# Seven block products for eight in the second product of a mixture layer's first stage, with one group of low parts made on GpSimd

## The chip, the core and the metric

The kernel runs on one core of one Trainium2 chip. The metric is the device time of one launch in microseconds, the median over several runs. The engines are TensorE (PE, with its weight loads listed as PEld), VectorE (DVE), ScalarE (ACT) and GpSimd (POOL); SyncE (SP) issues most transfers.

## The reference

Three stages follow each other. A retention layer gives 1536 tokens of 512 features. Layer 1 normalises them and passes them through a gated hidden layer of 1536. Layer 2 adds four experts of hidden size 1024, weighted by normalised probabilities.

```python
x = attn_out.transpose(0, 2, 1, 3).reshape(B * S, H * D)      # 1536 x 512
# layer 1
xn = x / sqrt(mean(x * x) + 1e-6) * rms_g
g, val = xn @ w_gate, xn @ w_val                                # 512 x 1536 each
x = (g * sigmoid(g) * val) @ w_out                              # 1536 x 512
# layer 2
p = domain_probs / (domain_probs.sum(-1, keepdims=True) + 1e-9)
out = sum(p[:, e:e + 1] * (maximum(x @ w1[e], 0) @ w2[e]) for e in range(4))
```

The product that the change touches is the last one of layer 1, hidden values times `w_out`.

## The kernel before

**Precision.** Every operand of a product is split into a high part (rounded to the format fp32r) and a low part (the rest, `raw - high`), and one product of two operands is three matmuls, high x high, low x high and high x low (`three`, L518 to L522).

**Tiling.** The tokens are two sets `j` of 768, each in two halves `a` of 384 (`TB`). A *unit* `q` is one pair of hidden blocks (gate and value, or two hidden blocks of an expert) for one set: a 2x2 block product of `x` (halves of the tokens, halves of the 512 features) with a 2x2 arrangement of weights. It is done with seven block products instead of eight (`PRODUCTS`, in the order M1, M5, M6, M2, M7, M4, M3), each two times three matmuls of 384 columns. Sums of weight blocks (`w_op`) and their parts are made on POOL, sums of token blocks on DVE or POOL. M6, M7 and M4 go on adding in the PSUM bank of M1, so ACT copies the bank after M1, M6 and M7 (`copy_up`), and the next of these products waits for the copy. DVE then forms the four results (`c11`, `c22_sum`, `c12`; the fourth lies in the bank).

**Layer 1** has 24 units (`Q1`), 12 hidden blocks for each of two sets. `silu` (ACT) and `hidden` (DVE, L975) make gate times value for the token half a=1 and then for a=0. In the kernel before, ACT rounds each (`hidden_hi`) into `h1_hi`, DVE subtracts (`hidden_lo`) into `h1_lo`, and four slots of these are held.

**The second product before.** For each pair of hidden blocks and each set (12 *rounds*; round r uses units 2r and 2r+1) there are eight tiles (`tile1`): four blocks of 128 output features times two token halves, each two hidden blocks times three matmuls of 384 columns. They go in turn to PSUM banks 6 and 7, and DVE adds each to `x_all` (`post1`, L1025). Tile n waits until tile n-2 is posted. The tiles are set by hand between the seven products of the two units that follow the round (`FIRST`, `SECOND`: how many at three places of a unit).

**Layer 2** has units of the same kind with `relu_hi`/`relu_lo` and output tiles `tile2`/`post2` of six matmuls of 512 columns. It is not changed but for addresses and for the units that overlap layer 1's last round.

**Queues.** The order of the work on each engine is written out by hand; each engine takes its queue in order, and semaphores with constant counts join them. DVE's order for a unit of layer 1 is posts, `c11`, posts, `c22_sum`, posts, `hidden(q,1)`, `c12`, `hidden(q,0)`, and two `hidden_lo`. POOL's order for one pair of blocks is `split_w(2p)`, `split_w(2p+1)`, `split_wd(p)`: for `w`, four sums of 256 elements a partition, one rounding of 1792 and seven subtractions of 256. `split_w_hi(c)` waits for the last unit that uses block c-2.

Of the kernel before, what the change touches and what calls it, by code (L numbers as in the profile page):

```python
# [32 lines left out]
J = 2  # L33
# [20 lines left out]

F1 = FF1 // P
# [29 lines left out]
def tiles_before(d):  # L85

    if d < F1 // 2:
        return 2 * T1N * (d + 1)
    return T1N * F1 + T2N * (last_unit(F1 + d - F1 // 2) - Q1 + 1)


def h_count(q):

    return 2 * q if q < Q1 else 2 * Q1 + 4 * (q - Q1)


def build(nc, qkv, wu, wd, small, t_y_decay, out):
# [3 lines left out]
    with ExitStack() as ctx:  # L101
        ctx.enter_context(nc.sbuf_tensor("arena", [P, 207 * 256 - 256], F32))

        def sem(name):
            return ctx.enter_context(nc.semaphore(name))

        X_HI, X_LO, ACC, W_RAW, W_HI, W_LO, WD, HH, HL, TMP, OWN = (
            o * KB for o in (17, 38, 101, 125, 133, 147, 161, 177, 189, 201, 219))
# [10 lines left out]
        wd_hi = [at(f"wd_hi{i}", [P, 2, DM], F32R, WD + 8 * KB * i) for i in range(2)]  # L119
        wd_lo = [at(f"wd_lo{i}", [P, 2, DM], F32R, WD + 8 * KB * i + 4 * KB) for i in range(2)]  # L120
        wd_raw = [at(f"wd_raw{i}", [P, 2, DM], F32, WD + 8 * KB * i + 4 * KB) for i in range(2)]
        h1_hi = at("h1_hi", [P, SLOTS1, 2, TB], F32R, HH)
        h1_lo = at("h1_lo", [P, SLOTS1, 2, TB], F32R, HL)
        h2_hi = at("h2_hi", [P, SLOTS2, 2, 2, TB], F32R, HH)
        h2_lo = at("h2_lo", [P, SLOTS2, 2, 2, TB], F32R, HL)
# [9 lines left out]
        y_decay = at("y_decay", [P, 2, DM], F32, HH)  # L135
        y_first = at("y_first", [P, DM], F32, TMP + 12 * KB)
        state = at("state", [P, B, PAIRS * DH], F32, HH + 4 * KB)
        guess = at("guess", [P, 2, TB], F32, HH + 6 * KB)
        guess_sq = at("guess_sq", [P, 2, TB], F32, HH + 9 * KB)
        squares = [at("squares0", [P, SPB, KT, CH], F32, WD + 8 * KB), at("squares1", [P, SPB, KT, CH], F32, HL + 6 * KB)]  # L140
# [51 lines left out]
        w_ready = sem("w_ready")  # L192
        wd_hi_ready = sem("wd_hi_ready")
# [47 lines left out]
        def _(sp):  # L241
# [33 lines left out]
            for p in range(1, F1 // 2):  # L275
# [22 lines left out]
        def _(pool):  # L298
# [88 lines left out]
            for n in range(NSTEP):  # L387
# [884 lines left out]
```

## Time and profile before

| | before |
|---|---|
| median of 3 runs | 844.63 us (844.29 to 844.9) |
| time of the profiled execution | 845.3 us |
| its span | 843.5 us |
| TensorE busy | 832.0 us (99%) |
| VectorE busy | 469.2 us (56%) |
| GpSimd busy | 408.1 us (48%) |
| ScalarE busy | 242.7 us (29%) |
| granted TensorE clock | 1.00 |

A busy share says how much of the span an engine had an instruction at work. TensorE's matmuls overlap, so the mean duration of one (335 ns) is longer than the distance between two; the work is counted by that distance. In the timelines a row is the start, the duration, the engine, the line and the operation, and in brackets the idle time before it and what ended it. A row with x2 or more covers neighbouring instructions together.

### The profile page before, as it was taken

How to read it: one execution, taken by the hardware profiler on the slowest of the kernel's cores; microseconds unless marked ns; L12 is line 12 of the kernel's file. 1: busy time of each engine (PE TensorE's matmuls, PEld its weight loads, DVE VectorE, ACT ScalarE, POOL GpSimd, SP SyncE). 2: the span in 40 equal slices, each digit the busy share in tenths (PEclk: the TensorE clock that was granted, in tenths of full speed). 3: DMA queues.
4: the chain of work that ended last, by engine and by line, in shares of the span. 5: the costliest groups of instructions: out<-in, count | busy, mean ns of one | idle time of the engine just before them, and what ended most of it. 6: DMA issues, size and time to landing. Idle time of an engine off the chain costs nothing.

```text
span 843.5 us, 12814 instructions
## 1 busy us (share of the span) xinstructions
PE 832.0 (99%) x4846; PEld 770.9 (91%) x4846; DVE 469.2 (56%) x776; ACT 242.7 (29%) x483; POOL 408.1 (48%) x460
## 2 busy tenths in 40 slices
PE   8999999999999999999999999999999999999998
PEld 7888999999999998889899989889899898898997
DVE  4698455545555558774554554545545545545545
ACT  2676222222322325422222222222212212222221
POOL 3998835546372739832836336336326325425100
PEclk9999999999999999999999999999999999999999
DMA  9801010100110010101101100110110110110003
GB/s 343 319 33 51 26 51 26 51 26 26 33 44 26 26 51 26 51 1 51 51 8 44 51 13 38 51 31 21 51 40 10 51 51 2 51 51 1 25 14 137
DMA packets 12876, 43.15 MB, mean 51 GB/s; under 512 B 1425, under 2 KB 1809, under 8 KB 12817
## 3 DMA queue, kind: packets, MB, share of 16 engines
q1 hardware_dynamic: 12528, 41.69, 14.0%
q8 instruction: 40, 0.66, 0.3%
q10 hardware_dynamic: 288, 0.65, 0.2%
q14 instruction: 20, 0.16, 0.1%
HBM read 39.19 MB, written 3.15 MB: 50 GB/s over the span
## 4 chain that ended last, share of the span: by engine, by line
PE 93%; POOL 2%; DMA 1%; DVE 1%; ACT 1%; issue 1%; SPq 0%; DVEq 0%
PE bank L520 30%; PE bank L521 30%; PE bank L522 30%; DMA ring<-qkv 1%; PE bank L469 1%; PE bank L462 1%; PE bank L449 1%; PE bank L499 1%; POOL w_lo L342 1%; POOL x_lo L237 0%; ACT x_hi L706 0%; DVE x_sum L233 0%; POOL wd_lo L361 0%; PE bank L482 0%; POOL squares L310 0%
## 5 line engine op out<-in xcount | busy, mean ns | idle before, releaser
L520 PE MATMUL bank<-x_hi,w_hi 128*128 128x384 f32 x784 | 263.9, 337 | 3.1 <-DVE x_lo L237 0.9
L522 PE MATMUL bank<-x_lo,w_hi 128*128 128x384 f32 x784 | 262.8, 335 | 0.0
L521 PE MATMUL bank<-x_hi,w_lo 128*128 128x384 f32 x784 | 262.8, 335 | 0.0
L1041 DVE SCALAR_TENSOR_TENSOR out_acc<-bank,p_norm,out_acc 128x512 f32<-128x512 f32 (+1 forms) x181 | 135.0, 746 | 127.7 <-PE bank L522 127.3
L520 PEld LDWEIGHTS bank<-x_hi,w_hi 128*128 128x128 f32 x784 | 147.2, 188 | 10.9 <-issue 5.5
L521 PEld LDWEIGHTS bank<-x_hi,w_lo 128*128 128x128 f32 x784 | 147.2, 188 | 5.5
L522 PE MATMUL bank<-wd_lo,h_hi 128*128 128x512 f32 (+1 forms) x386 | 152.0, 394 | 0.0
L521 PE MATMUL bank<-wd_hi,h_lo 128*128 128x512 f32 (+1 forms) x386 | 151.6, 393 | 0.0
L520 PE MATMUL bank<-wd_hi,h_hi 128*128 128x512 f32 (+1 forms) x386 | 149.9, 388 | 0.6 <-DVE out_acc L1037 0.3
L522 PEld LDWEIGHTS bank<-x_lo,w_hi 128*128 128x128 f32 x784 | 147.1, 188 | 0.0
L342 POOL TENSOR_TENSOR w_lo<-w_raw,w_hi 128x256 fp32r<-128x256 f32 x196 | 142.8, 762 | 3.0 <-ACT w_hi L678 0.8
L354 POOL TENSOR_SCALAR wd_hi<-wd_raw 128x1024 fp32r<-128x1024 f32 x21 | 22.1, 1053 | 213.5 <-DMA wd_raw<-wd 213.5
L711 ACT ACTIVATE u<-bank 128x384 f32<-128x384 f32 x112 | 55.1, 492 | 200.4 <-PE bank L522 200.3
L335 POOL TENSOR_SCALAR w_hi<-w_raw 128x1792 fp32r<-128x1792 f32 x26 | 44.4, 1707 | 126.4 <-PE bank L522 125.7
L313 POOL TENSOR_TENSOR w_raw<-w_raw 128x256 f32<-128x256 f32 x112 | 83.0, 763 | 19.9 <-DMA w_raw<-wu 17.7
L729 ACT ACTIVATE h_hi<-bank 128x384 fp32r<-128x384 f32 x96 | 47.3, 493 | 138.7 <-PE bank L522 64.8
L522 PEld LDWEIGHTS bank<-wd_lo,h_hi 128*128 128x128 f32 x386 | 72.4, 188 | 15.2
L520 PEld LDWEIGHTS bank<-wd_hi,h_hi 128*128 128x128 f32 x386 | 72.5, 188 | 13.1 <-issue 1.5
L521 PEld LDWEIGHTS bank<-wd_hi,h_lo 128*128 128x128 f32 x386 | 72.4, 188 | 11.9
L999 DVE SCALAR_TENSOR_TENSOR h_lo<-bank,h_hi 128x384 fp32r<-128x384 f32 x96 | 53.2, 554 | 43.6 <-ACT h_hi L729 43.6
L959 DVE TENSOR_TENSOR bank<-bank,m 128x384 f32<-128x384 f32 x56 | 31.6, 565 | 71.2 <-PE bank L522 71.2
L520 PE MATMUL bank<-h_hi,wd_hi 128*128 128x384 f32 x192 | 64.3, 335 | 1.1 <-DVE x_all L1025 1.1
(71 smaller groups left out, 874.5 us busy)
## 6 DMA issues: line engine op xcount, KB each, us to landing
w_raw<-wu SPq DMA_DIRECT2D x28, 512.0 KB, 4.3
ring<-qkv SPq DMA_DIRECT2D x23, 512.0 KB, 9.1
wd_raw<-wd SPq DMA_DIRECT2D x22, 512.0 KB, 3.5
out<-out_acc SPq DMA_DIRECT2D x11, 256.0 KB, 2.0
ring<-qkv ACTq DMA_DIRECT2D x1, 512.0 KB, 7.3
y_first<-t_y_decay SPq DMA_DIRECT2D x1, 256.0 KB, 8.0
out<-out_acc SPq DMA_DIRECT2D x2, 128.0 KB, 1.8
small_sb<-small ACTq DMA_DIRECT2D x1, 126.0 KB, 5.2
```

The source lines that it names most:

```text
L313: return nc.gpsimd.tensor_tensor(w_raw[:, WS[to], :, :], w_raw[:, WS[a], :, :], w_raw[:, WS[b], :, :], ALU.subtract).then_inc(w_sums, 1)
L335: nc.gpsimd.tensor_scalar(w_hi[c % 2][:, :, :, :], w_raw[:, 0:7, :, :], 1.0, 1.0, ALU.mult, ALU.mult).then_inc(w_hi_ready, 1)
L342: nc.gpsimd.tensor_tensor(w_lo[c % 2][:, WS[ws], :, :], w_raw[:, WS[ws], :, :], w_hi[c % 2][:, WS[ws], :, :].bitcast(F32), ALU.subtract).t ...
L354: nc.gpsimd.tensor_scalar(wd_hi[i][:, :, :], wd_raw[i][:, :, :], 1.0, 1.0, ALU.mult, ALU.mult).then_inc(wd_hi_ready, 1)
L520: pe.matmul(dst, s_hi, m_hi, start=first, stop=False, skip_group_check=True)
L521: pe.matmul(dst, s_lo, m_hi, start=False, stop=False, skip_group_check=True)
L522: return pe.matmul(dst, s_hi, m_lo, start=False, stop=last, skip_group_check=True)
L711: nc.scalar.activation(tile[:, s, :], bank[3 * s][:, 0:TB], ACT.Copy).then_inc(u_copied, 1)
L729: nc.scalar.activation(h2_hi[:, q % 2, v, a, :], src, ACT.Relu).then_inc(hi_ready, 1)
L959: nc.vector.tensor_tensor(bank[3 * s + 2][:, 0:TB], bank[3 * s + 2][:, 0:TB], m1[:, s, :], ALU.add).then_inc(c11_ready, 1)
L999: nc.vector.scalar_tensor_tensor(out=h2_lo[:, q % 2, v, a, :], in0=src, scalar=0.0, in1=h2_hi[:, q % 2, v, a, :].bitcast(F32), op0=ALU.max ...
L1041: nc.vector.scalar_tensor_tensor(out=to, in0=new, scalar=p, in1=to, op0=ALU.mult, op1=ALU.add).then_inc(posted, 1)
```

## The change

The hidden values of a round become a 2x2 block operand of their own: token halves a by the two hidden blocks v of units 2r and 2r+1. `w_out`'s two blocks by two halves of 256 features are the other operand. Seven products (`DOWNS`: M2, M1, M6, M7, M4, M5, M3) of two 128-feature tiles each replace the eight tiles: 14 tiles of three matmuls instead of eight of six. M6, M7, M4 add on in the banks of M1, and M3 in those of M5; the banks are posted after every product, so there are 14 posts a round instead of eight, and each tile waits for the post of tile n-2 as before.

`hidden` writes to SBUF (`h1_raw`, `h1_a21`). DVE makes four sums of hidden blocks (`hidden_sum`), ACT rounds them in four groups (one, two, two and two blocks of 384), and DVE subtracts for groups 0, 1 and 2; GpSimd does so for group 3 (S1 and S4) in rounds 0 to 9, and DVE in rounds 10 and 11. GpSimd makes four sums, one rounding of 1792 and seven subtractions of 256 for each `w_out` block pair, where it had one rounding of 1024 and two subtractions of 512. At the start ACT and DVE take these parts of the first block pair. The places of the tiles and the orders of all queues are new. The hidden operands take the place of the four slots in SBUF, and the second hidden buffer of layer 2 lies over them, so its first write waits for layer 1's last tile. `dynamic_dma_scratch_size=2048` is given to the program and the arena grows from 206 KB to 221 KB a partition.

```diff
+DOWNS = (("M2", "A12", "B21", True, ((0, 0),)), ("M1", "A11", "B11", True, ((0, 0),)),
+         ("M6", "S2", "T2", False, ((1, 0),)), ("M7", "S3", "T3", False, ((1, 1),)),
+         ("M4", "A22", "T4", False, ((0, 1),)), ("M5", "S1", "T1", True, ((1, 1),)),
+         ("M3", "S4", "B22", False, ((1, 0),)))
+HS = {"A12": 0, "A11": 1, "S2": 2, "S3": 3, "A22": 4, "S1": 5, "S4": 6}
+GROUPS = (slice(0, 1), slice(1, 3), slice(3, 5), slice(5, 7))
...
-T1N = 2 * KT
+T1N = 2 * NP
...
-FIRST, SECOND = (0, 1, 2), (2, 1, 2)
-EARLY, LATE = (0, 0, 2), (2, 2, 2)
-END0, END1 = (0, 2, 2), (2, 1, 1)
-NEXT0, NEXT1 = (0, 1, 2, 2), (3, 0, 0, 0)
+FIRST, SECOND = (0, 0, 0, 2, 2, 2, 0), (0, 2, 2, 2, 2, 0, 0)
+EARLY, LATE = (0, 0, 0, 0, 2, 2, 2), (0, 2, 2, 2, 2, 0, 0)
+END0, END1 = (0, 0, 0, 2, 2, 2, 2), (2, 2, 0, 0, 2, 0, 0)
+NEXT0, NEXT1 = (0, 0, 0, 0, 2, 2, 2), (2, 2, 2, 2, 0, 0, 0)
+TILES, TILES_NEXT = (0, 1, 0, 1, 2, 0, 2), (0, 0, 0, 0, 2, 0, 4)
...
 # GpSimd
+            def split_wd(d):
+                i = d % 2
+                sum_wd_13(d)
+                sum_wd_24(d)
+                pool.wait_ge(wd_sums, 4 * d + 4)
+                nc.gpsimd.tensor_scalar(wd_hi[i][:, :, :], wd_raw[i][:, 0:7, :], 1.0, 1.0,
+                                        ALU.mult, ALU.mult).then_inc(wd_hi_ready, 1)
+                pool.wait_ge(wd_hi_ready, d + 1)
+                for _, _, ws, _, _ in DOWNS:
+                    nc.gpsimd.tensor_tensor(wd_lo[i][:, WS[ws], :], wd_raw[i][:, WS[ws], :],
+                                            wd_hi[i][:, WS[ws], :].bitcast(F32), ALU.subtract).then_inc(wd_ready, 1)
...
+            sum_w(2)
+            hidden_lo(0, 3)
+            for p in range(1, D1):
+                split_w_hi(2 * p)
+                split_w_lo(2 * p)
                 split_w(2 * p + 1)
+                hidden_lo(2 * p - 1, 3)
                 split_wd(p)
+                if p < D1 - 1:
+                    sum_w(2 * p + 2)
+                    hidden_lo(2 * p, 3)
...
 # TensorE
+            def down1(r, i):
+                n, p, s = T1N * r + i, r // J, i % 2
+                _, xs, ws, first, _ = DOWNS[i // 2]
+                pe.wait_ge(wd_ready, wd_count(p, i // 2))
+                pe.wait_ge(hid_split[GROUP_OF[xs]], r + 1)
+                if n == 0:
+                    pe.wait_ge(x_normal, 16)
+                elif n >= 2:
+                    pe.wait_ge(posted, n - 1)
+                c = slice(P * s, P * s + P)
+                mm = three(bank[6 + s][:, 0:TB], wd_hi[p % 2][:, WS[ws], c], wd_lo[p % 2][:, WS[ws], c],
+                           h1_hi[:, HS[xs], :], h1_lo[:, HS[xs], :], first, True)
...
 # ScalarE
+            def hidden_hi(r, g):
+                act.wait_ge(hid_sums, 4 * r + (2 if g == 2 else 4))
+                nc.scalar.activation(h1_hi[:, GROUPS[g], :], h1_raw[:, GROUPS[g], :], ACT.Copy).then_inc(hid_hi_ready[g], 1)
...
             def unit1(q):
+                r = q // 2 - 1
+                if q % 2 == 0:
+                    hidden_hi(r, 0)
+                    hidden_hi(r, 1)
                 copy_up(q, "M6", u2)
+                if q % 2 == 0:
+                    hidden_hi(r, 2)
                 silu(q, 0)
                 copy_up(q, "M7", u3)
+                if q % 2 == 0:
+                    hidden_hi(r, 3)
                 silu(q, 1)
-                hidden_hi(q, 1)
-                if q + 1 < Q1:
-                    copy_up(q + 1, "M1", m1)
-                hidden_hi(q, 0)
+                copy_up(q + 1, "M1", m1)
...
 # VectorE
+            def hidden_sum(r, to):
+                a21, a11, a12, a22 = (h1_a21[:, :] if n == "A21" else h1_raw[:, HS[n], :] for n in ("A21", "A11", "A12", "A22"))
+                s1, s2 = h1_raw[:, HS["S1"], :], h1_raw[:, HS["S2"], :]
+                x, y, op, of, count = {"S3": (a11, a21, ALU.subtract, hid_ready, 2), "S1": (a21, a22, ALU.add, hid_ready, 3),
+                                       "S2": (s1, a11, ALU.subtract, hid_sums, 2),
+                                       "S4": (a12, s2, ALU.subtract, hid_ready, 4)}[to]
...
+            def first1(q):
+                r = q // 2 - 1
+                hidden_lo(r, 0)
+                hidden_lo(r, 1)
+                c11(q)
+                post1(r, 0, 2)
+                hidden_lo(r, 2)
+                c22_sum(q)
+                post1(r, 2, 4)
                 hidden(q, 1)
+                post1(r, 4, 6)
                 c12(q)
                 hidden(q, 0)
+            def second1(q):
+                r = q // 2 - 1
+                post1(r, 6, 8)
+                hidden_sum(r + 1, "S3")
+                post1(r, 8, 10)
+                c11(q)
+                post1(r, 10, 13)
+                c22_sum(q)
+                post1(r, 13, 14)
+                hidden(q, 1)
+                hidden_sum(r + 1, "S1")
+                hidden_sum(r + 1, "S2")
+                c12(q)
+                hidden(q, 0)
+                hidden_sum(r + 1, "S4")
...
-    nc = bacc.Bacc("TRN2", target_bir_lowering=False, num_devices=1)
+    nc = bacc.Bacc("TRN2", target_bir_lowering=False, num_devices=1, dynamic_dma_scratch_size=2048)
```

## Rows read from the trace of the kernel before

**Rows 1.** The page: span, and busy time by engine.
```profile
span 843.5 us, 12814 instructions
PE 832.0 (99%) x4846; PEld 770.9 (91%) x4846; DVE 469.2 (56%) x776; ACT 242.7 (29%) x483; POOL 408.1 (48%) x460
```

**Rows 2.** The page: the chain that ended last, by engine.
```profile
PE 93%; POOL 2%; DMA 1%; DVE 1%; ACT 1%; issue 1%; SPq 0%; DVEq 0%
```

**Rows 3.** Busy time by stretch: start:end length, engines (instructions), clock, DMA share, GB/s.
```profile
54.00:86.00 32.00, 29.92 (x157) 26.97 (x157) 26.00 (x42) 21.60 (x40) 29.44 (x29) 1.00 0.10 33
86.00:320.00 234.00, 234.00 (x1352) 234.00 (x1351) 121.71 (x226) 68.19 (x143) 120.20 (x144) 1.00 0.11 35
320.00:368.00 48.00, 45.55 (x239) 41.44 (x238) 40.45 (x55) 20.57 (x35) 39.24 (x35) 1.00 0.10 33
368.00:843.00 475.00, 472.64 (x2355) 424.83 (x2354) 247.63 (x396) 103.58 (x209) 179.98 (x206) 1.00 0.11 37
```

**Rows 4.** Groups of instructions from 86 to 320 us: count, busy us, mean ns, idle before.
```profile
L522 PE MATMUL bank<-h_lo,wd_hi 128*128 128x384 f32 x168 | 56.1, 334 | 0.0
...
L342 POOL TENSOR_TENSOR w_lo<-w_raw,w_hi 128x256 fp32r<-128x256 f32 x74 | 51.8, 737 | 0.9
...
L313 POOL TENSOR_TENSOR w_raw<-w_raw 128x256 f32<-128x256 f32 x41 | 29.4, 738 | 18.3 <-DMA w_raw<-wu 17.5
...
L335 POOL TENSOR_SCALAR w_hi<-w_raw 128x1792 fp32r<-128x1792 f32 x11 | 18.8, 1705 | 80.1 <-PE bank L522 79.5
```

**Rows 5.** Timeline of DVE around one unit's end.
```profile
199.95 0.56 DVE L988 TENSOR_TENSOR bank<-c,bank 128x384 f32<-128x384 f32 x1 [0.99 <-ACT bank L721]
200.48 0.57 DVE L973 TENSOR_TENSOR bank<-bank,u 128x384 f32<-128x384 f32 x1
201.15 0.57 DVE L988 TENSOR_TENSOR bank<-bank,gate 128x384 f32<-128x384 f32 x1
201.62 0.55 DVE L993 TENSOR_TENSOR h_lo<-bank,h_hi 128x384 fp32r<-128x384 f32 x1
...
203.60 0.56 DVE L1025 TENSOR_TENSOR x_all<-bank,x_all 128x384 f32<-128x384 f32 x1 [0.61 <-PE bank L522]
```

**Rows 6.** Timeline of PE: the last matmul of the tile posted at 203.60.
```profile
203.23 0.33 PE L522 MATMUL bank<-h_lo,wd_hi 128*128 128x384 f32 x1
```

**Rows 7.** Timeline of ACT: one silu of a=1, and two neighbouring instructions.
```profile
211.92 0.48 ACT L721 ACTIVATE bank<-bank 128x384 f32<-128x384 f32 x1 [2.63 <-PE bank L522]
...
214.00 0.49 ACT L711 ACTIVATE m<-bank 128x384 f32<-128x384 f32 x1 [0.48 <-PE bank L522]
214.39 0.49 ACT L725 ACTIVATE h_hi<-bank 128x384 fp32r<-128x384 f32 x1
```

**Rows 8.** The chain that ended last, 339 to 342 us: start, us, what.
```profile
340.36 0.56 DVE x_all L1025
340.91 0.14 issue
341.05 0.41 PE bank L520
```

**Rows 9.** Timeline of PE: the second matmul after that wait.
```profile
341.30 0.34 PE L521 MATMUL bank<-h_hi,wd_lo 128*128 128x384 f32 x1
```

**Rows 10.** The tile of token sums, whole span: count, duration min/median/max in ns.
```profile
L706 ACT ACTIVATE x_hi<-x_sum x16: 828/844/854, 50.0 to 362.0; 128x768 fp32r<-128x768 f32 x16
L237 DVE TENSOR_TENSOR x_lo<-x_sum,x_hi x13: 941/1117/1530, 53.3 to 366.1; 128x768 fp32r<-128x768 f32 x13
L233 DVE TENSOR_TENSOR x_sum<-x_all x6: 991/1397/1739, 48.8 to 355.3; 128x768 f32<-128x768 f32 x6
L237 POOL TENSOR_TENSOR x_lo<-x_sum,x_hi x6: 992/1012/1017, 59.7 to 82.6; 128x384 fp32r<-128x384 f32 x6
```

**Rows 11.** Timeline of DVE, one token sum.
```profile
320.67 1.51 DVE L233 TENSOR_TENSOR x_sum<-x_all 128x768 f32<-128x768 f32 x1
```

**Rows 12.** Timeline of POOL at the same time.
```profile
321.33 2.86 POOL L342 TENSOR_TENSOR w_lo<-w_raw,w_hi 128x256 fp32r<-128x256 f32 x2
```

More of the change, by code:

```diff
@@ L202, in build @@
         hid_ready = sem("hid_ready")
+        hid_sums = sem("hid_sums")
+        hid_hi_ready = [sem(f"hid_hi_ready{g}") for g in range(len(GROUPS))]
+        hid_split = [sem(f"hid_split{g}") for g in range(len(GROUPS))]
         hi_ready = sem("hi_ready")
@@ L626, in _, with unit @@
-            unit1(4 * end + 2, None, (end, 0, 0), END0)
-            unit1(4 * end + 3, None, (end, 0, sum(END0)), END1)
-            def unit2(q, k=None, first=0, counts=(0, 0, 0, 0), tiles=(1, 1, 2, 2)):
-                f, j = UNITS2[q - Q1]
-                c = F1 + f
-                def some(place):
-                    for i in range(sum(counts[:place]), sum(counts[:place + 1])):
-                        tile1(end, 1, first + i)
+            def unit(q, k=None, r=None, first=0, downs=(0,) * NP, tiles=(0,) * NP):
+                c, j = UNITS1[q] if q < Q1 else (F1 + UNITS2[q - Q1][0], UNITS2[q - Q1][1])
+                for place in range(NP):
+                    product(q, c, j, k, PRODUCTS[place][0])
+                    if q == 0 and place == 0:
+                        sum_squares(2)
+                    elif q == 0 and place == 2:
+                        sum_squares(3)
+                    for i in range(sum(downs[:place]), sum(downs[:place + 1])):
+                        down1(r, first + i)
@@ L652, in _ @@
-            unit2(Q1, 2, 0, NEXT0, (0, 0, 0, 0))
-            unit2(Q1 + 1, None, sum(NEXT0), NEXT1, (0, 2, 2, 2))
+            unit(0, 0)
+            unit(1)
+            unit(2, 1, 0, 0, EARLY)
+            unit(3, None, 0, sum(EARLY), LATE)
+            for r in range(1, F1 - 2):
+                unit(2 * r + 2, None, r, 0, FIRST)
+                unit(2 * r + 3, None, r, sum(FIRST), SECOND)
+            unit(Q1 - 2, None, F1 - 2, 0, END0)
+            unit(Q1 - 1, None, F1 - 2, sum(END0), END1)
@@ L654, in _ @@
+            unit(Q1, 2, F1 - 1, 0, NEXT0)
+            unit(Q1 + 1, None, F1 - 1, sum(NEXT0), NEXT1, TILES_NEXT)
             for q in range(Q1 + 2, NQ):
-                unit2(q, 3 if q == Q1 + 2 else None)
+                unit(q, 3 if q == Q1 + 2 else None, tiles=TILES)
             for i in range(T2N - 1):
@@ L800, in _ @@
                     make_y_decay(4)
+                elif n == 7:
+                    split_wd_hi(0)
                 elif n == 8:
@@ L1127, in _ @@
             hidden(1, 1)
+            hidden_sum(0, "S3")
+            hidden_sum(0, "S1")
+            hidden_sum(0, "S2")
             c12(1)
             hidden(1, 0)
[L1130 to L1140 removed]
@@ L1141, in _ @@
-            unit1(4 * end + 2, (end, 0, 0), END0)
+            hidden_sum(0, "S4")
+            split_wd_lo_t(0)
+            hidden_lo(0, 0)
+            c11(2)
+            hidden_lo(0, 1)
+            c22_sum(2)
+            post1(0, 0, 2)
+            hidden_lo(0, 2)
+            hidden(2, 1)
+            post1(0, 2, 4)
+            c12(2)
+            hidden(2, 0)
+            post1(0, 4, 6)
+            second1(3)
+            for r in range(1, F1 - 2):
+                first1(2 * r + 2)
+                second1(2 * r + 3)
@@ L1142, in _ @@
+            r = F1 - 2
+            q = Q1 - 2
+            hidden_lo(r, 0)
+            hidden_lo(r, 1)
+            c11(q)
+            post1(r, 0, 2)
+            hidden_lo(r, 2)
+            c22_sum(q)
+            post1(r, 2, 4)
+            hidden(q, 1)
+            post1(r, 4, 6)
+            c12(q)
+            hidden(q, 0)
+            hidden_lo(r, 3)
+            post1(r, 6, 8)
             q = Q1 - 1
-            post1(end, 0, 4)
-            post1(end, 0, 5)
+            post1(r, 8, 10)
```

374 lines of the change are left out of this document (171 added, 203 removed).

## The prediction

> **What bounds the kernel now.** I read the busy shares first: TensorE is at work in 832.0 of 843.5 us, VectorE in 56% and GpSimd in 48% [rows 1]. The chain that ended last says the same: 93% of it is TensorE [rows 2]. The table by stretch says where this is so. From 86 to 320 us, layer 1's steady part, TensorE is never idle and issues 1352 matmuls in 234.0 us, one each 0.1731 us. In this stretch VectorE is busy 121.7 of 234 us and GpSimd 120.2. Before it, from 54 to 86 us, and after it, from 320 to 368 us where layers 1 and 2 meet, TensorE is idle 2.1 and 2.45 us, and here VectorE (26.0 of 32, 40.5 of 48) and GpSimd (29.4 of 32) are nearly full. In layer 2 TensorE is idle 2.4 of 475 us. The clock is 1.00 throughout [rows 3]. So a matmul taken out is worth its whole distance, as long as VectorE's and ScalarE's answers still come in time.
>
> **What it removes.** Each of 12 rounds loses 48 - 42 = 6 matmuls of 384 columns. The group's mean of 334 ns [rows 4] is not the price, since they overlap; the distance is: 72 x 0.1731 = 12.5 us. A round of two units then takes (84 + 42) x 0.1731 = 21.8 us where it took 22.9. One product is 6 matmuls (1.04 us), one of the new tiles 3 (0.52 us).
>
> **What it adds on VectorE.** For a round: 14 posts for 8, four sums, and low parts of five blocks in three instructions for four of one block. An instruction with an operand in PSUM lasts 0.56 us, and the next can start 0.47 later, or 0.67 later if it waits for that result [rows 5]. For 384 elements with both inputs in SBUF there is no row: 768 elements take 0.94 to 1.74 us [rows 10]; I take 0.54 for 384 (between half of 0.94 and 0.56) and, in both cases, a next start 0.07 before the end. The excess over 0.94 is GpSimd: the sum at 320.67 took 1.51 us while two GpSimd instructions that last 0.74 took 2.86 together [rows 4, 11, 12]. I add 0.2 us to a short instruction and 0.41 to a long one where GpSimd is at work; 0 and 0.8 are the bounds. In all a round holds 14 x 0.47 + 6 x 0.5 + 4 hidden x 0.5 + 4 x 0.55 + about 2.8 = 17 of 21.8 us. VectorE is not the bound by that, but it has little slack when an answer is due, so I follow the queues.
>
> **One steady round.** Time 0 is the end of the previous unit's M3. A result is seen 0.20 us after its last matmul's slot (203.23 + 0.17 to 203.60) [rows 5, 6]. ScalarE needs 0.48 for 384 elements (next start after 0.39) and 0.84 for 768 [rows 7, 10]. When TensorE waited for VectorE, its matmul started 0.14 after the post's end, and the next 0.25 instead of 0.17 later, so a late answer costs its end + 0.21 [rows 8, 9].
> The chain to the first tile, with GpSimd quiet: M4 ends at -1.04, silu to -0.36, `hidden(1)` starts at -0.33, sum S1 0.27, S2 0.84, `c12` 1.31, `hidden(0)` 1.97, S4 2.57 to 3.11 (about 0.6 where one waits for its own result). ScalarE's rounding of group 0 waits for S4, though it does not need it: 3.14 to 3.63. The low part of group 0 is done at 4.20, so TensorE can start at 4.41. It is due after four products, at 4.16: **0.25 late**. VectorE goes on: low parts of group 1 from 4.40 (0.87), `c11` 5.27, post 0 from 5.74 to 6.30, just at the limit for tile 2 (which waits for tile 0's post); then post 1, low parts of group 2, `c22_sum`, post 2 to 8.58, so tile 4 starts at 8.79 instead of 8.59: **0.2 late**. Together 0.47 us.
> With GpSimd in S1 and S2 the whole chain starts 0.4 later: 0.9 us. With GpSimd in the low parts of groups 1 and 2 too: 1.7 us. Which it is follows from GpSimd's queue. For even rounds GpSimd has finished the weights' sums about 2 us into the unit and then waits for group 3's high parts (7 to 8 us in): 0.9. For odd rounds it goes from sums to the rounding and to seven subtractions of `w_lo`, from about 4 to 9 us: 1.7. In the second unit I find nothing late: the first of its tiles comes after two products, and VectorE waits there, not TensorE. Rounds 1 to 9: 5 x 1.7 + 4 x 0.9 = **12.1 us**, which is the whole saving.
>
> **GpSimd.** In two rounds: three times (4 x 0.72 + 1.71 + 7 x 0.70 = 9.5), for two `w` and one `w_out` pair, four subtractions of 384 (1.01 each), and the wait for a `w_raw` transfer (17.5 us over five pairs, 3.5): 36 us of 43.6 [rows 4, 10]. VectorE's SBUF instructions add some 5. It fits, and group 3 is due 6 us into the second unit, after GpSimd's queue has reached it.
>
> **Where the layers meet.** Round 10 has its first unit like the others, and also two tiles after M3 and two after the next M1, with VectorE between them busy with two `hidden` values and group 3: 1.3 us for the first unit. Then VectorE's queue for the next three units, in distances: posts 0.47, `c` 0.47, token sums and their low parts of 768 elements 1.2 (the medians, less the overlap) [rows 10], output posts 0.66. It comes to 15.0 + 11.9 + 20.3 = 47.2 us, against 10.4 + 10.4 + 19.8 = 40.6 us of TensorE. The same count for the kernel before is 38.5 against 42.7, and TensorE was idle 2.45 us there [rows 3]. So VectorE becomes the bound here: at least 6.6 - 2.45 = 4 us more than before. Following the waits one by one as above gave 10 us of stalls, 7.6 more than before. I take **6 us**, and 2 and 8 as bounds.
>
> **The start.** VectorE and GpSimd are almost full from 54 to 86 us [rows 3]. VectorE gets two subtractions for the first `w_out` pair (768 and 1024 elements, some 2 us) and four sums, and loses four low parts (1.9 us). GpSimd has 2.9 us of sums where it had 2.6 of low parts. The last wait in that stretch ended with a GpSimd low part of x, and this is pushed back by ScalarE's new rounding ahead of S4's. I take 1.5 us; bounds 0 and 3.
>
> **At no cost.** Layer 2's places and waits are as before; the write of its second hidden buffer must wait for tile 13 of round 11, which ends 2.1 us after M2 of that unit, while ScalarE's next copy (M7) is ready only 3.1 us after it. If that cover were gone it would cost ScalarE 1 us once. The transfers have the same bytes. ScalarE is a third full and hidden behind VectorE except in the chain above, where it is counted.
>
> **Sum.** -12.5 + 12.1 + 1.3 + 6 + 1.5 = +8.4 us. On the profiled execution's 845.3 us that is 853.7; its span is 1.8 us shorter than its time, and the time is 0.7 above the median, so against the median it is **853.0 us**.
>
> **A rule beside a row.** VectorE's x_sum took from 0.99 to 1.74 us, 0.4 more at the median than at the least [rows 10]. The Trainium skill, SBUF — State Buffer, section Who interferes with whom, says that VectorE instructions with two SBUF inputs contend with GpSimd for a shared port pair, and that it is an exclusive lock: the loser waits for the other's whole instruction. By it a short instruction would lose as much as a long one, so cutting the work in blocks of 384 would pay more often. That is the second rival.
>
> **Rivals.** (1) *The chain keeps up.* If GpSimd's work does not fall on the sums and low parts, a round loses 0.47 us, ten of them 4.7; with 2 us where the layers meet and 0.5 at the start it gives 844.6 - 12.5 + 7.2 = 839.3 us, faster. It decides at about 0.7 us of stall a round. For it: ideal lateness is only 0.25 + 0.2 us, each at the limit of what the rows resolve. Against it: GpSimd is busy 36 of 43.6 us, and VectorE's queue at the junction is too long without it. (2) *Each short SBUF instruction loses 0.45 us*, the median excess of long ones: S1 and S2 lose 0.5 more a round, nine rounds 4.5 us: 857.5 us. (3) *GpSimd becomes the bound*: if its 36 us grow past 45 (the same excess of 0.7 us on each of 14 VectorE instructions in two rounds), `w_hi` comes late by some 3 us in each of five pairs: 868 us. For it: two GpSimd instructions in 2.86 us; against: nine idle microseconds before it matters. (4) *All is hidden*: 844.6 - 12.5 = 832 us.
>
> **How the numbers follow.** No change can be told below 0.2% (1.7 us). Forecast, 848 to 856: 0.44. Rival 2 and its like, 856 to 862: 0.16. Rival 3: 0.10. Between forecast and rival 1, 843 to 846.4: 0.09, and just above, 846.4 to 848: 0.03. Rival 1: 0.15. Rival 4: 0.03. Slower: 0.73, same 0.09, faster 0.18. The range of 8 in 10 leaves out rivals 3 and 4 and the better part of rival 1: 841 to 862. The likeliest case's own range is 848 to 856.
>
> **What would show it.** Right: 504 matmuls of tiles for 576 at the same distance; between 86 us and the last rounds TensorE idle before the first tile (released by DVE h_lo) and before tiles 2 and 4 (DVE x_all), 0.5 to 1.7 us a round, more in odd rounds; rounds of 22.7 and 23.5 us; where the layers meet 8 to 9 us of idle TensorE with VectorE without a gap. Wrong: rounds of 21.8 to 22.3 us (rival 1), short sums of 0.9 us and more (rival 2), TensorE waiting for POOL w_lo (rival 3).

## The result: 3.9% slower

The changed kernel takes 877.3 us (876.37 to 879.17, 4 runs) against 844.76 us (844.29 to 844.92), a ratio of 1.0387 with a 95% interval of 1.0374 to 1.04. The direction was forecast; the size was not: 853.0 us was the forecast and 862 the upper end, and even the slowest rival, 868 us, lies below the result.

The page of the changed kernel: span, busy time by engine, and the chain that ended last.

```profile
span 875.0 us, 13005 instructions
...
PE 835.1 (95%) x4774; PEld 765.8 (88%) x4774; DVE 562.6 (64%) x888; ACT 253.0 (29%) x483; POOL 481.9 (55%) x527
...
PE 79%; DVE 9%; issue 4%; POOL 4%; DMA 2%; ACT 1%; SPq 1%; DVEq 0%
```

TensorE issues 72 matmuls fewer than before, but it now holds 79% of the chain where it held 93% [rows 1, 2]; VectorE has come in with 9%. Busy time by stretch shows where TensorE lost it (length, then PE, PEld, DVE, ACT and POOL with instructions, clock, DMA share, GB/s):

```profile
54.00:86.00 32.00, 24.93 (x124) 21.72 (x123) 30.25 (x40) 19.75 (x36) 28.30 (x25) 0.97 0.10 33
...
150.00:170.00 20.00, 16.97 (x96) 16.10 (x95) 16.71 (x25) 6.04 (x11) 19.50 (x21) 1.00 0.08 27
170.00:190.00 20.00, 19.73 (x113) 19.13 (x112) 14.90 (x28) 7.01 (x13) 10.95 (x15) 1.00 0.08 27
...
350.00:370.00 20.00, 15.26 (x70) 12.87 (x68) 18.64 (x27) 7.27 (x14) 15.92 (x14) 0.91 0.00 0
370.00:390.00 20.00, 15.51 (x75) 13.96 (x76) 18.81 (x27) 7.67 (x13) 13.32 (x10) 0.95 0.16 53
...
430.00:875.00 445.00, 442.11 (x2204) 397.41 (x2202) 231.95 (x371) 96.97 (x195) 173.10 (x198) 1.00 0.11 37
```

The start (54 to 86 us) and the meeting of the layers (350 to 390 us) have VectorE above 90% and TensorE at three quarters. In the steady part good and bad stretches alternate, and the bad one has GpSimd at 19.5 of 20 us. Layer 2 is as before. The clock is no longer 1.00 throughout.

The starts of each unit's first matmul in the timeline of PE give the sums (us, differences of starts; "work saved" is the matmuls taken out at their distance of 0.1731, negative where tiles were moved forward; the last column is the lengthening plus the work saved):

| units | before | after | work saved | new idle and slow time |
|---|---|---|---|---|
| start of unit 3 | 84.84 | 91.26 | -1.0 | 5.4 |
| units 3 to 21 (rounds 1 to 9) | 219.44 | 230.29 | 11.4 | 22.3 |
| units 22 to 25 | 58.24 | 72.33 | 2.1 | 16.2 |
| the rest | | +0.1 | 0 | 0.1 |

That is 44.0 - 12.5 = 31.5 us, the difference of the spans. By the two pages TensorE is idle 39.9 us for 11.5 before, 28.4 more; in the other 15.6 us of the 44.0 it counts as busy, at a lower clock or just after a wait. In the steady part every second unit takes 11.44 us, its work and nothing more. All is lost in the first units, whose work is 10.40 us: 13.12, 11.52, 14.19, 11.15, 14.25, 11.13, 14.77, 10.92 and 14.84 us for rounds 1 to 9. Even rounds lose 0.8 on the average, odd ones 3.8.

### The profile page after: what moved, and what is told of

It is laid out like the page before. It is cut to its first block, busy times and chain, and to the rows that moved or that the text cites. A ratio compares the mean times of both kernels' runs of the same rounds, so it can differ in the third digit from the quotient of the medians.

```text
span 875.0 us, 13005 instructions
## 1 busy us (share of the span) xinstructions
PE 835.1 (95%) x4774; PEld 765.8 (88%) x4774; DVE 562.6 (64%) x888; ACT 253.0 (29%) x483; POOL 481.9 (55%) x527
## 4 chain that ended last, share of the span: by engine, by line
PE 79%; DVE 9%; issue 4%; POOL 4%; DMA 2%; ACT 1%; SPq 1%; DVEq 0%
PE bank L593 26%; PE bank L594 26%; PE bank L595 26%; DMA ring<-qkv 2%; DVE h_raw L1043 1%; DVE x_lo L269 1%; DVE h_lo L1047 1%; POOL w_lo L378 1%; DVE x_all L1091 1%; POOL x_lo L269 1%; DVE h_raw L1031 1%; POOL ring L339 1%; DVE bank L1016 1%; POOL squares L346 1%; DVE c L1009 0%
## 5 line engine op out<-in xcount | busy, mean ns | idle before, releaser
L378 POOL TENSOR_TENSOR w_lo<-w_raw,w_hi 128x256 fp32r<-128x256 f32 x196 | 155.7, 829 | 3.0 <-ACT w_hi L713 0.8
L419 POOL TENSOR_SCALAR wd_hi<-wd_raw 128x1024 fp32r<-128x1024 f32 x16 | 17.6, 1098 | 203.8 <-DMA wd_raw<-wd 203.8
L349 POOL TENSOR_TENSOR w_raw<-w_raw 128x256 f32<-128x256 f32 x112 | 87.3, 800 | 20.1 <-DMA w_raw<-wu 17.9
L1091 DVE TENSOR_TENSOR x_all<-bank,x_all 128x384 f32<-128x384 f32 x152 | 80.1, 551 | 24.7 <-PE bank L595 24.6
L593 PEld LDWEIGHTS bank<-wd_hi,h_hi 128*128 128x128 f32 x386 | 73.1, 189 | 16.2 <-issue 4.4
L595 PEld LDWEIGHTS bank<-wd_lo,h_hi 128*128 128x128 f32 x386 | 72.9, 189 | 15.4
L593 PE MATMUL bank<-h_hi,wd_hi 128*128 128x384 f32 x168 | 59.8, 356 | 25.3 <-issue 14.5
L594 PEld LDWEIGHTS bank<-wd_hi,h_lo 128*128 128x128 f32 x386 | 72.9, 189 | 12.1
```

The costliest lines, as they stand in the source:

```text
L349: return nc.gpsimd.tensor_tensor(w_raw[:, WS[to], :, :], w_raw[:, WS[a], :, :], w_raw[:, WS[b], :, :], ALU.subtract).then_inc(w_sums, 1)
L378: nc.gpsimd.tensor_tensor(w_lo[c % 2][:, WS[ws], :, :], w_raw[:, WS[ws], :, :], w_hi[c % 2][:, WS[ws], :, :].bitcast(F32), ALU.subtract).t ...
L419: nc.gpsimd.tensor_scalar(wd2_hi[i][:, :, :], wd2_raw[i][:, :, :], 1.0, 1.0, ALU.mult, ALU.mult).then_inc(wd_hi_ready, 1)
L593: pe.matmul(dst, s_hi, m_hi, start=first, stop=False, skip_group_check=True)
L594: pe.matmul(dst, s_lo, m_hi, start=False, stop=False, skip_group_check=True)
L595: return pe.matmul(dst, s_hi, m_lo, start=False, stop=last, skip_group_check=True)
```

## What happens in an odd round

Round 3, whose first unit begins at 150.22 us. VectorE's timeline (start, duration):

```profile
150.48 0.96 DVE L1043 TENSOR_TENSOR h_raw<-h_a,h_raw 128x384 f32<-128x384 f32 x1
151.48 0.98 DVE L1043 TENSOR_TENSOR h_raw<-h_raw 128x384 f32<-128x384 f32 x1
152.38 0.55 DVE L1016 TENSOR_TENSOR bank<-bank,u 128x384 f32<-128x384 f32 x1
153.04 0.56 DVE L1031 TENSOR_TENSOR h_raw<-bank,gate 128x384 f32<-128x384 f32 x1
153.63 1.62 DVE L1043 TENSOR_TENSOR h_raw<-h_raw 128x384 f32<-128x384 f32 x1
155.84 2.51 DVE L1047 TENSOR_TENSOR h_lo<-h_raw,h_hi 128x384 fp32r<-128x384 f32 x2 [0.59 <-ACT h_hi L761]
```

GpSimd's timeline at the same time:

```profile
149.60 3.46 POOL L349 TENSOR_TENSOR w_raw<-w_raw 128x256 f32<-128x256 f32 x4 [3.47 <-DMA w_raw<-wu]
153.15 1.70 POOL L371 TENSOR_SCALAR w_hi<-w_raw 128x1792 fp32r<-128x1792 f32 x1
154.93 6.82 POOL L378 TENSOR_TENSOR w_lo<-w_raw,w_hi 128x256 fp32r<-128x256 f32 x7
```

And the first tile on TensorE ("issue": the profile names nothing that it waited for; VectorE's low part of group 0 had ended 0.10 us before):

```profile
157.04 0.41 PE L593 MATMUL bank<-h_hi,wd_hi 128*128 128x384 f32 x1 [2.49 <-issue]
```

Sum S4 (153.63) is two SBUF inputs of 384 elements, an instruction that takes 0.56 us when nothing hinders it. It took 1.62. GpSimd's rounding had begun at 153.15 and ended at 154.85; S4 ended 0.40 after that. S1 and S2 took 0.96 and 0.98 over GpSimd's sums, the low parts after them 1.1 and 1.5 over its subtractions, and those seven took 6.8 us where they take 4.9 alone. The operations with a PSUM operand, in between, took their 0.55. All that is left of the other engine's instruction enters, here 1.22 us, and not a share of it: in the prediction I had allowed S4 nothing for the rounding. The low part of group 0 shows it on a small scale: it began 0.04 us after a subtraction of 0.73 us and ended 0.41 us after that one's end.

Round 1 is the other way about. There the rounding began 4.24 us into the unit, after S4, and S4 took 0.56 us; instead the low part of group 1 (768 elements, 0.96 alone) met the rounding and took 2.20. In rounds 3, 5, 7 and 9 the rounding began 2.9 to 3.0 us into the unit and S4 took 1.61 or 1.62.

The Trainium skill, SBUF — State Buffer, section Who interferes with whom, says that a VectorE instruction with two SBUF inputs contends with a GpSimd instruction that reads SBUF for a shared port pair and that the loser fully blocks. These rows agree: S4 took 1.62 us and ended 0.40 us after the rounding.

## The experiments

Six of the runs have one time each: e1, e2, e3 and e6 stand beside 845.16 us for the kernel before on the same chip, e5 and e4 beside 844.69. The four times of the changed kernel lie 2.8 us apart, so the main readings of these six are the lengths of units in their traces. "First units" are those of rounds 1 to 9. "Port theory" and "chain theory" are what the first expectation calls so.

### e1_pool_waits

```diff
-                split_w(2 * p + 1)
+                sum_w(2 * p + 1)
+                pool.wait_ge(hid_split[1], 2 * p)
+                split_w_hi(2 * p + 1)
+                split_w_lo(2 * p + 1)
```

> Port theory (VectorE's instructions with two SBUF inputs are held for the whole of a GpSimd instruction; in odd rounds the 1.70 us rounding of w_hi meets sum S4 and the seven w_lo meet the low parts): with GpSimd's rounding held back until the low parts of group 1 are done, odd rounds' first units take 11.2 to 12.2 us instead of 13.1 to 14.8, even ones stay at 11.0 to 11.5, and the kernel gains 9 to 15 us (862 to 868). Chain theory (the chain of sum, rounding and low part is too long by itself, GpSimd has no part in it): odd rounds stay above 13 us and the time is within 2 us of the changed kernel, or worse by the w parts that come later.

Measured: 872.4 us. In the odd rounds from 3 on S4 fell from 1.62 us to 0.56 (0.66 once). Odd first units, which had taken 13.1 to 14.8 us, take 11.8 to 12.1: the held instructions are what made them long. But even first units rose from 11.1 to 12.4: GpSimd's next work now fell on their sums and low parts (S2 0.98, the low parts of groups 0 and 1 1.11 and 1.49). The port theory named the direction and the size for the odd rounds and missed that the collision would move; the gain was 5 us and not 9 to 15.

### e2_pool_narrow

```diff
+                k = slice(0, 8 if narrow[0] else P)
-                return nc.gpsimd.tensor_tensor(w_raw[:, WS[to], :, :], w_raw[:, WS[a], :, :], w_raw[:, WS[b], :, :],
+                return nc.gpsimd.tensor_tensor(w_raw[:, WS[to], :, k], w_raw[:, WS[a], :, k], w_raw[:, WS[b], :, k],
```

and likewise in `split_w_hi` and `split_w_lo`. Most columns of these weight parts are left stale, so what this kernel puts out is not the layers' result; it serves for its time alone.

> GpSimd's sums, roundings and subtractions of the layers' first weights are done on 8 of each 128 columns from block 2 to block 13, so the rest of these parts is left stale; VectorE, ScalarE and TensorE do what they did. Port theory: what is left in a round is the chain with a quiet GpSimd, 0.5 to 0.9 us a round in odd and even rounds alike (w_out's parts are still made), 22 us of stalls in rounds 1 to 9 become 5 to 9, and where the layers meet 20 us of stalls become 12 to 16; 852 to 860 us. Chain theory: odd rounds keep 3.8 us of stall, time within 3 us of the changed kernel.

Measured: 853.89 us. Every first unit from round 2 on takes 10.92 to 10.96 us, odd and even alike: 0.53 us of stall where the prediction's chain with a quiet GpSimd had 0.47. Its operations on the hidden values, from 100 to 310 us (count, duration min/median/max in ns):

```profile
L1054 DVE TENSOR_TENSOR h_lo<-h_raw,h_hi x28: 558/951/979, 108.0 to 309.9; 128x768 fp32r<-128x768 f32 x18, 128x384 fp32r<-128x384 f32 x10
L1050 DVE TENSOR_TENSOR h_raw<-h_raw x20: 557/559/919, 105.1 to 308.3; 128x384 f32<-128x384 f32 x20
...
L1050 DVE TENSOR_TENSOR h_raw<-h_a,h_raw x10: 558/558/559, 104.5 to 306.0; 128x384 f32<-128x384 f32 x10
```

and the same groups in the changed kernel:

```profile
L1047 DVE TENSOR_TENSOR h_lo<-h_raw,h_hi x27: 558/1098/2195, 106.8 to 304.8; 128x768 fp32r<-128x768 f32 x18, 128x384 fp32r<-128x384 f32 x9
L1043 DVE TENSOR_TENSOR h_raw<-h_raw x18: 557/975/1624, 103.5 to 298.8; 128x384 f32<-128x384 f32 x18
...
L1043 DVE TENSOR_TENSOR h_raw<-h_a,h_raw x9: 557/762/1075, 103.0 to 295.5; 128x384 f32<-128x384 f32 x9
```

So in rounds 1 to 9 GpSimd's weight work cost 22.3 - 5.0 = 17.3 us (some 1.1 of it by way of the clock, see below), and the chain itself 5.0.

Units 22 to 25 fell from 72.3 to 65.6 us: of the 16.2 lost there 9.5 remain. The other 6.7 are not all collisions. 3.0 of them lie in unit 25, whose one long wait lasts 3.45 us here and 3.44 in the changed kernel; what differs there is the clock, which fell in the changed kernel and not here. The 3.7 of units 22 to 24 are collisions together with one more fall of the clock, and these were not separated.

### e3_a12_early

```diff
-                act.wait_ge(hid_sums, 4 * r + (2 if g == 2 else 4))
+                if g == 0:
+                    act.wait_ge(hid_ready, 4 * r + 4)
+                else:
+                    act.wait_ge(hid_sums, 4 * r + (3, 2, 4)[g - 1])
```

VectorE's low parts of groups 0 and 1 wait for S4 themselves instead.

> ScalarE rounds group 0 (A12) as soon as hidden(q,0) is written, not after sum S4. Port theory and chain theory both say that S4 stands in VectorE's queue ahead of the low part, so only ScalarE's 0.5 us leaves the chain: first units shorter by 0.3 to 0.6 us each, 3 to 6 us in all (871 to 874). If S4's place in ScalarE's wait were the main cause, odd rounds would fall by 1.6 us or more (865 or less).

Measured: 872.01 us. First units are shorter by 5.8 us in all; those of rounds 3, 5, 7 and 9 still take 13.4 to 13.6: S4 still takes 1.62 us and stands in VectorE's queue ahead of the low part. The gain is about what ScalarE's half microsecond is worth; it is largest, 1.2 and 1.4 us, in rounds 7 and 9, where the clock of the changed kernel fell and this one's did not.

### e6_lo3_on_dve

```diff
 # GpSimd
-                hidden_lo(2 * p - 1, 3)
-                    hidden_lo(2 * p, 3)
 # VectorE, at the end of first1
                 hidden(q, 0)
+                hidden_lo(r, 3)
```

> Group 3's low parts are made on VectorE in every round, after the first unit's hidden(q,0), as rounds 10 and 11 do; GpSimd loses 2 us a round. VectorE is waiting there, so by port theory it costs nothing there and GpSimd's next work comes 2 us earlier: within 2 us of the changed kernel. If GpSimd's share in the hidden values were what makes the kernel slow, it would gain 5 us or more; if VectorE's load were, it would lose 5 us or more.

Measured: 872.5 us, 4.8 less than the changed kernel. The port theory's "within 2 us" was missed, and the 5 us of its rival just not reached; that VectorE's load makes the kernel slow is ruled out. First units are 3.7 us shorter in all. In rounds 3, 5, 7 and 9 they take 13.4 to 13.6 us: the rounding now begins 3.6 to 3.8 us into the unit, after S4, so S4 lasts 0.65, and the low part of group 0 meets it instead and takes 1.36. Making group 3's low parts on GpSimd, the change's own feature, did not pay: it relieved VectorE in a place where VectorE was waiting.

### e5_short_rounding

```diff
-                nc.gpsimd.tensor_scalar(w_hi[c % 2][:, :, :, :], w_raw[:, 0:7, :, :], 1.0, 1.0,
-                                        ALU.mult, ALU.mult).then_inc(w_hi_ready, 1)
+                for i in range(7):
+                    hi = nc.gpsimd.tensor_scalar(w_hi[c % 2][:, i, :, :], w_raw[:, i, :, :], 1.0, 1.0,
+                                                 ALU.mult, ALU.mult)
+                hi.then_inc(w_hi_ready, 1)
```

> The changed kernel with GpSimd's rounding of w as seven instructions of 256 elements in place of one of 1792; the same elements are read and written. If VectorE's instruction is held until the end of the GpSimd instruction under way (port held by instruction), S4 in odd rounds falls from 1.62 us to 0.7 to 0.9, odd first units from 14.2 to about 13.4, and the kernel by 2 to 5 us. If the two engines only share bandwidth, S4 stays at 1.6 us and the kernel is the same or up to 3 us slower, for GpSimd's extra instructions.

Measured: 866.83 us, 10.5 less, twice what the port theory expected at most. Odd first units are down to 11.4, even ones up to 12.6. It isn't a clean test of the length alone: GpSimd's queue grew, and in odd rounds the rounding then began after S4 (4.24 us into the unit for 2.9), which alone would have taken S4 to 0.56. So the expected 0.7 to 0.9 for an S4 beside short roundings was not tested. VectorE in round 3 (whose first unit begins at 150.35 us):

```profile
153.34 0.56 DVE L1045 TENSOR_TENSOR h_raw<-h_raw 128x384 f32<-128x384 f32 x1
154.49 0.56 DVE L1049 TENSOR_TENSOR h_lo<-h_raw,h_hi 128x384 fp32r<-128x384 f32 x1 [0.59 <-ACT h_hi L763]
155.22 0.96 DVE L1049 TENSOR_TENSOR h_lo<-h_raw,h_hi 128x768 fp32r<-128x768 f32 x1 [0.17 <-ACT h_hi L763]
```

and GpSimd:

```profile
154.59 2.23 POOL L372 TENSOR_SCALAR w_hi<-w_raw 128x256 fp32r<-128x256 f32 x3
```

Here VectorE began both times before the rounding that it met (154.49 before 154.59, 155.22 before 155.28) and took 0.56 and 0.96, its undisturbed times. It is GpSimd that lost: its three roundings took 0.72, 1.17 and 0.41, where one takes 0.40 alone. In these rows, as in those of round 3, who begins first decides who pays.

### e4_steady

All at once: the wait of e1, ScalarE's early rounding of e3, the low parts of e6, and `hidden(q,0)` before S2.

```diff
                 hidden(q, 1)
                 hidden_sum(r + 1, "S1")
-                hidden_sum(r + 1, "S2")
                 c12(q)
                 hidden(q, 0)
+                hidden_sum(r + 1, "S2")
                 hidden_sum(r + 1, "S4")
```

> Together: GpSimd's rounding of the odd weight block waits for the low parts of group 1, ScalarE rounds A12 at once, VectorE makes hidden(q,0) before sum S2, and group 3's low parts are VectorE's. Port theory: the chain to the first tile is now within its 4.16 us when GpSimd is quiet, and about 0.5 late when it is at work; first units of 10.5 to 11.5 us in rounds 1 to 9 (13.1 to 14.8 in the odd ones before), so 12 to 18 us less than the changed kernel: 860 to 865. Start and meeting of the layers are nearly as before. Chain theory with GpSimd of no weight: the reorder alone gives 0.5 us a round, 870 or more.

Measured: 862.84 us. First units take 10.8 to 11.3 us, 7.1 us of stall in nine rounds for 22.3. The start and units 22 to 25 are no better (unit 3 begins at 92.3 for 91.3, the four units take 72.9 for 72.3). In unit 22, which takes 15.8 us for 14.0, GpSimd's work on the first weights of layer 2 (`wd_hi`, `wd_lo`), which nothing holds back, fall on S2, S4 and the low part of group 0: 1.43, 1.46 and 1.43 us for 0.56.

### e7_edges_old

```diff
+OLD = (0, 1, F1 - 2, F1 - 1)
+def base(r):
+    return sum(8 if i in OLD else T1N for i in range(r))
...
+                if r in OLD:
+                    d, a = TILES1[i]
...
+                    for v in range(2):
+                        k = ((4, 5), (0, 6))[d // 2][v]
+                        hi, lo = h_old(2 * r + v, a)
+                        mm = three(bank[6 + s][:, 0:TB], wd_hi[p % 2][:, k, c], wd_lo[p % 2][:, k, c], hi, lo,
+                                   v == 0, v == 1)
```

The orders of the queues for these rounds are those of the kernel before; the addresses, the arena and `dynamic_dma_scratch_size` are those of the changed kernel.

> Rounds 0, 1, 10 and 11 as in the kernel before (eight tiles, hidden values kept in PSUM), rounds 2 to 9 with seven products as in e4_steady. Theory (the losses at the start and where the layers meet come from VectorE's longer queue there): units 0 to 3 and 22 to 25 take what they take in the kernel before; 48 matmuls, 8.3 us, are saved, and rounds 2 to 9 lose 0.2 to 1 us each: 838 to 845 us, faster than the kernel before. Rival (the losses at the edges come from the layout, the smaller scratch or the new waits): the edges stay 5 us or more above the kernel before, 848 or more.

Measured: 842.75 us, 0.9978 of the kernel before (0.9968 to 0.9988): 0.2% less, clear of 1 but so small that it counts as the same time. Unit 3 begins at 84.41 (84.84 before) and units 22 to 25 take 58.24 us, to the hundredth what they take before. So the losses at both edges come from the new form of these rounds with its queues, and neither from the addresses nor the smaller scratch. What in the new form costs most, VectorE's longer queue or the collisions, this run does not tell. First units of rounds 3 to 9 still take 11.1 to 11.3.

### e9_held and e8_held_short

```diff
+                if p >= 2:
+                    pool.wait_ge(hid_split[1], 2 * p - 3)
                 split_w(2 * p)
-                sum_w(2 * p + 1)
-                if 2 <= p < D1:
+                sum_w_13(2 * p + 1)
+                if p >= 2:
                     pool.wait_ge(hid_split[1], 2 * p - 2)
+                sum_w_24(2 * p + 1)
                 split_w_hi(2 * p + 1)
```

> e7_edges_old, with two of GpSimd's sums for the odd weight block and all four for the next pair's first block held back until VectorE has made the low parts of group 1. Port theory: nothing of GpSimd falls on S1, S2, S4 and the low parts of groups 0 and 1 in either kind of round, so these last 0.56 and 0.95 us and first units fall from 11.1 to 11.3 us to 10.4 to 10.9; 2.5 to 6 us less than e7_edges_old: 837 to 840. If the remaining 0.85 us a round is VectorE's own queue, nothing moves (842 to 844), or the weights come late and TensorE waits for w_lo.

`hid_split[1]` counts VectorE's low parts of group 1. Measured: 838.69 us, 0.993 (0.9914 to 0.9947), the fastest version here, though still less than 2% below the kernel before. First units of rounds 2 to 9 take 10.41 to 10.76 us. Not every collision is gone: in rounds 4, 6 and 8 S4 still lasts 0.91 us, in rounds 5, 7 and 9 S1 0.80 to 0.88. Its steady part, what follows, and layer 2:

```profile
84.00:310.00 226.00, 225.84 (x1294) 223.81 (x1294) 173.40 (x304) 74.43 (x141) 158.53 (x182) 1.00 0.11 36
310.00:357.00 47.00, 44.61 (x237) 40.99 (x236) 38.53 (x54) 21.22 (x37) 42.80 (x39) 1.00 0.10 34
357.00:837.00 480.00, 477.33 (x2379) 429.01 (x2377) 252.35 (x402) 104.50 (x211) 180.07 (x207) 1.00 0.11 37
```

VectorE is busy 77% of the steady part (52% in the kernel before), and TensorE is idle 0.16 of 226 us: VectorE's load is not what held TensorE there.

`e8_held_short` adds e5's short roundings.

> e9_held with the rounding of w as seven instructions of 256. It holds VectorE's low parts of group 2 for 0.4 us at most, where one of 1792 can hold them for 1.7; but GpSimd's queue grows by 1.5 us a block. Port theory: within 1.5 us of e9_held, on either side. If GpSimd's queue is the next bound, 3 us or more slower, with TensorE waiting for w_lo.

Measured: 842.14 us, 0.9973 (0.9962 to 0.9984), 3.5 us slower than e9_held. By the number the expectation's second case came, but not by its way. The view of TensorE's waits from 130 to 300 us names GpSimd:

```profile
PE bank L636 <- POOL wd_lo L461: 1.4, 3, 0.5
```

The timelines of TensorE, VectorE and GpSimd at one of the three, in round 4:

```profile
169.72 0.41 PE L636 MATMUL bank<-h_hi,wd_hi 128*128 128x384 f32 x1 [0.46 <-POOL wd_lo L461]
168.71 1.78 DVE L1119 TENSOR_TENSOR h_lo<-h_raw,h_hi 128x384 fp32r<-128x384 f32 x2
167.13 2.07 POOL L461 TENSOR_TENSOR wd_lo<-wd_raw,wd_hi 128x256 fp32r<-128x256 f32 x2
```

GpSimd's subtraction had ended at 169.20. The last to come was VectorE's low part of group 0, the first of the x2: it ended at 169.62, 0.10 us before the matmul, and had taken 0.91 us beside that subtraction. So GpSimd's longer queue brings the collisions back: the low part of group 0 takes 0.91 us in rounds 4, 6 and 8 (0.56 in e9_held), S2 0.91 to 1.08 in rounds 3, 5, 7 and 9 (0.55 to 0.66), and first units are 2.35 us longer in all. GpSimd itself comes late once, where the layers meet: its low part of x for unit 24 makes TensorE wait 1.3 us. With GpSimd held back already, short instructions cost more than they gave.

## Why the prediction was right and wrong

**Right: the saving and the chain.** 72 matmuls at 0.1731 us, 12.5 us; second units lose nothing; the first tile is late by the chain hidden, sum, rounding, low part, and the later ones by posts queued behind it. With a quiet GpSimd the size was right too, 0.53 us for 0.47 (e2), and in even rounds 3.1 us in four for 3.6.

**Wrong: odd rounds.** The term "5 x 1.7" measured 19.2 us, not 8.5. The step that failed is the price of a contended instruction, "I add 0.2 us to a short instruction and 0.41 to a long one", with 0.8 as the bound. It was read from x_sum [rows 10], whose GpSimd neighbours were instructions of 0.7 to 1 us, and carried over to a place where the neighbour is a rounding of 1.70 us. With it went the overlap: the prediction put the rounding and the subtractions "from about 4 to 9 us", behind S4 (2.57 to 3.11), and added nothing to S4 and to the low part of group 0; in rounds 3, 5, 7 and 9 the rounding began at 2.9 to 3.0, before S4. S4 lost 1.06, S1 and S2 0.4 each, the low parts 0.5 each: 2.9 us in round 3, and 3.4 with the 0.47 of the quiet chain, for 3.8 measured. Rival 2 named the mechanism, and its sign, short sums of 0.9 us and more, came; its price of 0.45 an instruction, again a median over short neighbours and given to S1 and S2 alone, was too small: 857.5 us.

The right price stood in the trace of the kernel before. VectorE's longest x_sum, and what GpSimd did beside it:

```profile
349.13 1.74 DVE L233 TENSOR_TENSOR x_sum<-x_all 128x768 f32<-128x768 f32 x1
349.05 1.01 POOL L237 TENSOR_TENSOR x_lo<-x_all,x_hi 128x384 fp32r<-128x384 f32 x1
```

The subtraction had begun 0.08 us earlier and had 0.93 us left; x_sum lost 0.80 against the 0.94 that 768 elements take at least. The bound of 0.8 was what is left of a neighbour of 1.01 us, and no bound beside one of 1.70.

**Wrong: where the layers meet.** "I take 6 us" (after 1.3 for round 10's first unit) measured 16.2 in all. The bounds were 2 and 8, and my own count wait by wait had given more than the value that I took. The step that failed is the value put on the stalls there, counted from VectorE's queue in undisturbed or median distances and at a clock of 1.00. e2 splits the 16.2: 9.5 remain with VectorE's longer queue and whatever collides with GpSimd's low parts of x there, 3.0 are the clock in unit 25, and 3.7 are collisions and another fall of the clock. What the 9.5 consist of stays open. One wait is a matter of order (e2 keeps it, the old form in e7 does not have it): TensorE stood 3.4 us for the first-time post of an output tile, which stood behind a token sum of 1.65 us and two low parts in VectorE's queue. The changed kernel's waits, largest first (us in total, times, longest):

```profile
PE bank L593 <- issue: 14.5, 10, 2.6
PE bank L593 <- DVE x_all L1091: 5.7, 9, 1.2
PE bank L593 <- DVE wd_lo L1056: 3.8, 1, 3.8
PE bank L593 <- DVE out_acc L1103: 3.4, 1, 3.4
```

"issue" are the waits for the first tile of a round: each of the ten ended 0.10 us after one of VectorE's low parts. The row tells the time and not the cause.

**Wrong: the start.** "I take 1.5 us", bounds 0 and 3, measured 5.4. VectorE was to get 2 us of subtractions for the first `w_out` pair; they took 1.80 and 1.22 us, three of the four sums between them 0.90, 1.25 and 1.37 (0.56 alone), and the first tile stood 3.8 us behind the second. So part of it is the same price set too low, in a stretch with no slack, and up to 1.5 us are the clock; e7 removed all of it, but with the whole new form of these rounds, so the parts are read from the trace and not tested.

**Left out: the clock.** The prediction took 1.00 throughout. The granted clock of five stretches of the changed kernel:

```profile
84.60:87.60 3.00, 2.98 (x10) 3.00 (x11) 3.00 (x6) 1.83 (x4) 3.00 (x3) 0.51 0.00 0
252.00:260.00 8.00, 6.42 (x28) 6.45 (x29) 6.73 (x9) 4.32 (x8) 8.00 (x9) 0.79 0.10 18
300.00:308.00 8.00, 5.80 (x24) 5.83 (x25) 7.02 (x10) 4.09 (x7) 7.41 (x8) 0.79 0.01 2
356.00:361.00 5.00, 3.88 (x12) 3.56 (x12) 4.63 (x5) 3.14 (x6) 4.83 (x4) 0.66 0.01 2
388.00:395.00 7.00, 6.37 (x17) 5.24 (x18) 3.69 (x6) 0.00 (x0) 4.75 (x6) 0.52 0.00 0
```

Each time TensorE had stood for 1.9 to 3.8 us within one wait, and then went at its lower level (1.2 GHz) for 3 to 7 us, its matmuls of 384 columns 0.32 us apart instead of 0.17. TensorE was at work for 19.25 us of these stretches, so the clock cost 9.6 us at most, as an estimate. A part of it is won back, since VectorE catches up meanwhile: the first units of rounds 7 and 9 took 0.5 and 0.6 us more than that of round 5, where the clock did not fall. Rounds 3 and 5 had waits of 2.49 and 2.55 us without a fall, round 7 one of 2.56 with one, so the wait's length alone does not tell; what does stays open.

**Rivals.** Rival 1 (839.3 us) did not come; its stall of 0.47 us a round did in e2, where its condition held, but the start and the meeting of the layers kept e2 at 853.9. That e9_held takes 838.7 is luck as far as the number goes: it has the new form in eight rounds alone, saves 8.3 us and not 12.5, and loses next to nothing at the edges. Rival 3 (GpSimd the bound) was wrong here: from 86 to 320 us TensorE never waits for GpSimd in the view of its waits; in e8 there is one such wait, 1.3 us where the layers meet. Rival 4 (all hidden, 832 us) did not come.

## What to carry to other kernels

When work is moved to VectorE instructions with two SBUF inputs, list which GpSimd instruction can stand beside each, and take the whole of the longest one as the bound of the wait, not a mean of rows with other neighbours. Then follow GpSimd's queue as closely as VectorE's: a hold or a shorter instruction moves the collision to another place before it removes it (e1, e5, e6, e8). Holding GpSimd back by one more semaphore wait, and one placed earlier, until the short chain is over was worth 4 us here in eight rounds, without any work removed; moving two subtractions to GpSimd to relieve VectorE cost about 4.8. And a form that pays in the steady part need not be used in the rounds at the edges, where the queues are full: there the old form, with eight matmuls for each seven, was the faster by 20 us (e7_edges_old against e4_steady).

## What was not expected of the hardware

A VectorE instruction of 0.56 us with two SBUF inputs was held to 1.62 us by one GpSimd rounding of 1.70 us that had begun 0.48 us earlier, and three GpSimd roundings of 0.40 us took 2.23 us when VectorE had begun first; VectorE instructions of 384 elements with an operand in PSUM stayed at 0.54 to 0.57 us beside all of it. After single idle stretches of TensorE of 1.9 to 3.8 us its clock stood at half for 3 to 7 us in five places, and in two more with a wait of 2.5 us it did not fall.
